# Expert products on two blocks of 768 tokens instead of three of 512

## The reference

```python
def _moe2_ref(x, w_gate, w1, w2) -> np.ndarray:   # x 1536x320, E = 8 experts, F = 1024
    logits = x @ w_gate
    logits = logits - logits.max()
    P = np.exp(logits)
    for _ in range(8):
        P /= P.sum(1, keepdims=True) + 1e-09
        P /= P.sum(0, keepdims=True) + 1e-09
        P *= N / E
    for e in range(E):
        h = np.maximum(x @ w1[e], 0.0)
        ye = h @ w2[e]
        out += P[:, e:e + 1] * ye
    return out
```

## Time and profile before

| | us |
|---|---|
| median of 3 runs | 947.43 |
| the three runs | 945.85, 947.43, 947.50 |
| the profiled execution, its own time | 945.77 |
| its span on the page | 944.1 |
| PE busy | 933.1 (99%) |
| DVE busy | 648.5 (69%) |
| POOL busy | 440.4 (47%) |
| ACT busy | 353.0 (37%) |
| step 0 of the experts starts at | 266.85 |

### The profile page before, as it was taken

One profiled execution on the slowest core, in us unless ns is written; L12 is line 12 of the kernel. 1 busy time (PEld: TensorE's weight loads), 2 busy tenths in 40 slices (PEclk: granted clock), 3 DMA queues, 4 the chain that ended last, 5 costly groups with the idle time before them and its releaser, 6 DMA issues.

```text
span 944.1 us, 16696 instructions
## 1 busy us (share of the span) xinstructions
PE 933.1 (99%) x6519; PEld 889.8 (94%) x6529; DVE 648.5 (69%) x1066; ACT 353.0 (37%) x659; POOL 440.4 (47%) x501
## 2 busy tenths in 40 slices
PE   8999999999999999999999999999999999999998
PEld 5999888888789999999999999999999999999998
DVE  6787555458778899876666766666676666667664
ACT  5664543353453333333322432333243233323221
POOL 4463231057498646465733652573365256336000
PEclk9999999999999999999999999999999999999999
DMA  7980221011011111112111121111112111110000
GB/s 128 216 139 1 78 79 35 1 34 34 1 34 34 35 35 34 35 34 59 44 34 35 37 65 35 32 37 34 35 38 64 35 34 35 35 34 1 28 29 29
DMA packets 82796, 42.39 MB, mean 45 GB/s; under 512 B 54270, under 2 KB 82302, under 8 KB 82718
## 3 DMA queue, kind: packets, MB, share of 16 engines
q1 hardware_dynamic: 82510, 41.23, 17.0%
q10 hardware_dynamic: 208, 0.11, 0.1%
HBM read 39.13 MB, written 2.11 MB: 44 GB/s over the span
## 4 chain that ended last, share of the span: by engine, by line
PE 91%; DVE 6%; ACT 1%; issue 1%; POOL 0%; DVEq 0%; POOLq 0%; ACTq 0%
PE psB L1641 11%; PE psB L1642 11%; PE psB L1643 11%; PE psA L1627 8%; PE psA L1626 8%; PE psA L1625 8%; PE psA L1624 8%; PE psA L1554 8%; PE psB L1473 2%; PE psA L1452 2%; PE psB L1573 2%; PE psB L1575 2%; PE psB L1574 2%; DVE gl L1377 1%; PE psB L1580 1%
## 5 line engine op out<-in xcount | busy, mean ns | idle before, releaser
L676 POOL TENSOR_TENSOR wst<-raw_w,wst 128x128 fp32r<-128x128 f32 (+2 forms) x192 | 163.1, 862 | 304.1 <-ACT wst L891 175.3
L1641 PE MATMUL psB<-w2s,gh 128*128 128x320 f32 x768 | 238.6, 311 | 0.9 <-DVE acc L1351 0.9
L1643 PE MATMUL psB<-w2s,gl 128*128 128x320 f32 x768 | 237.3, 309 | 0.0
L1642 PE MATMUL psB<-w2s,gh 128*128 128x320 f32 x768 | 237.3, 309 | 0.0
L1377 DVE SCALAR_TENSOR_TENSOR gl<-part,gh 128x512 fp32r<-128x512 f32 x192 | 160.5, 876 | 63.4 <-ACT gh L998 62.8
L998 ACT ACTIVATE gh<-part 128x512 fp32r<-128x512 f32 x192 | 110.8, 624 | 245.3 <-DVE part L1371 245.3
L1627 PE MATMUL psA<-xop,wst 96*128 96x256 f32 x672 | 190.2, 283 | 0.0
L1626 PE MATMUL psA<-xop,wst 128*128 128x256 f32 x672 | 190.2, 283 | 0.0
L1625 PE MATMUL psA<-xop,wst 128*128 128x256 f32 x672 | 190.2, 283 | 0.0
L1624 PE MATMUL psA<-xop,wst 128*128 128x256 f32 x672 | 190.0, 283 | 0.0
L1641 PEld LDWEIGHTS psB<-w2s,gh 128*128 128x128 f32 x768 | 144.6, 188 | 1.3 <-DVE gl L1377 1.1
(11 more groups left out here) (193 smaller groups left out, 1377.3 us busy)
## 6 DMA issues: line engine op xcount, KB each, us to landing
raw_w<-in_moe_w_dram SPq DMA_DIRECT2D x32, 320.0 KB, 3.2
raw_w<-in_moe_w_dram SPq DMA_DIRECT2D x32, 256.0 KB, 2.7
raw_w<-in_moe_w_dram SPq DMA_DIRECT2D x96, 64.0 KB, 2.5
qs<-in_q_dram SPq DMA_DIRECT2D x12, 160.0 KB, 3.5
ks<-in_k_dram SPq DMA_DIRECT2D x12, 160.0 KB, 3.7
vz<-in_v_dram SPq DMA_DIRECT2D x12, 160.0 KB, 3.5
og<-in_o_gate_dram SPq DMA_DIRECT2D x12, 160.0 KB, 4.0
out_dram<-acc SPq DMA_DIRECT2D x5, 320.0 KB, 2.3
```

The source lines that it names most:

```text
L676: return pool.tensor_tensor(dst, raw, high.bitcast(F32), ALU.subtract)
L1641: pe.matmul(bank, gh[:, slot, cols], w2[:, f, 0, :], start=first, stop=False)
L1642: pe.matmul(bank, gh[:, slot, cols], w2[:, f, 1, :], start=False, stop=False)
L1643: last = pe.matmul(bank, gl[:, slot, cols], w2[:, f, 0, :], start=False, stop=end)
```

## The change

The experts take two blocks of WB = 768 tokens (halves of HT = 384), so there are 64 steps instead of 96 and a product is four matmuls of 384 columns. The seven products take turns in two banks of `psA`; the second projection has six token tiles, in the other two banks of `psA` and the four of `psB`, and its 36 matmuls are put in six pieces of six between the products. DVE adds each product by itself (six additions, `ADDS` = 6), and the two hidden tiles are finished at different points of the step. Weight slots are five: pair 0 alternates between two, pairs 1 to 3 have one each. The rounds stand at steps 4 to 11. The MLP still works on 512-token blocks; its middle block is half of either expert block, so the pieces of `xop` are 256, 128 and 384 columns a half, and step 0 needs the first two. The order of preparation changes to fit.

```diff
-    PREP = [0, 2, 1, 3]
+    PREP = [0, 1, 2, 3]
-    ROUND_AT = [5, 6, 7, 9, 10, 11, 13, 14]
+    ROUND_AT = [4, 5, 6, 7, 8, 9, 10, 11]
+    TOP_AT, MAX_AT = 2, 3
...
+        product_ps = lambda n, i: psA[:, (NPROD * n + i) % HB, 0:HT]
+        out_ps = lambda j: psA[:, HB + j, 0:DM] if j < HB else psB[:, j - HB, 0:DM]
...
         def slot_of(s, p):
-            return 2 * (s % 2) + p // 2 if p % 2 == 0 else 4 + p // 2
+            return s % 2 if p == 0 else 1 + p
...
# POOL
             pair_low(HALVES, 0)
-            pair_low(HALVES, 2)
-            rest_high(0)
+            kept_high(0)
             main_sums(0)
             main_lows(0)
             main_sums(1)
-            rest_high(1)
+            kept_high(1)
+            main_lows(1)
             pair_low(HALVES, 1)
+            pair_low(HALVES, 2)
+            kept_high(2)
             pair_low(HALVES, 3)
-            main_lows(1)
-            main_sums(2)
-            rest_high(2)
-            pair_low(HALVES + 1, PREP[0])
             main_lows(2)
...
# ACT, middle(n), between keep_first(n) and high_of(n, 0)
+                if n == 0:
+                    pair_s_high(s, 1)
+                    pair_w2_high(s, 2)
+                    pair_w1_high(s, 3)
+                if n == 1:
+                    pair_s_high(s, 2)
+                    x2_rest_high(2)
+                if n == 2:
+                    x2_high(2)
+                    pair_s_high(s, 3)
+                if at == 0 and n > 0:
+                    pair_s_high(s, 1)
+                    both_high(s, 2)
                 if at == 1 and n > 1:
+                    pair_s_high(s, 2)
+                    both_high(s, 3)
+                if at == 2 and n > 2:
                     pair_s_high(s, 3)
+                if s + 1 < STAGES:
+                    if at == 3:
+                        both_high(s + 1, 0)
+                    if at == 4:
+                        pair_s_high(s + 1, 0)
+                    if at == 7:
+                        both_high(s + 1, 1)
...
# DVE, pair(n)
+                if n > 0:
+                    low_of(n - 1, 1)
+                if n == 1:
+                    x2_rest_both(2)
+                    x2_rest_sums(2)
...
+                add(n, 1, part[:, 0, :], part[:, 4, :], 0)
+                if k is not None:
+                    if k == 0:
+                        dve.wait_ge(p_exp, 1)
+                    norm_rows(k)
+                add(n, 2, part[:, 2, :], part[:, 4, :], 0)
+                if p == 1 and blk > 0:
+                    for j in range(4, WT):
+                        read_o(blk - 1, j)
+                if k is not None:
+                    read_columns(k)
+                add(n, 3, part[:, 3, :], part[:, 2, :], 2)
+                if k is not None:
+                    norm_columns(k)
+                add(n, 4, part[:, 1, :], part[:, 3, :], 3)
+                add(n, 5, part[:, 2:4, :], part[:, 2:4, :], 4)
+                low_of(n, 0)
+                add(n, 6, part[:, 2, :], part[:, 2, :], 5)
+                if n == 1:
+                    x2_rest_low(2)
+                    dve.wait_ge(xa, XA * 2 + 1)
+                    sums_of_main(dve, xw, 0, 2)
+                if p == 0 and blk > 0:
+                    if blk == 1:
+                        dve.wait_ge(xl, XL * 3)
+                    for j in range(4):
+                        read_o(blk - 1, j)
...
# PE, pair(n)
+                at_least(pe, added, ADDS * n - 1)
+                product(n, 0, 0, 0)
+                if n == 1:
+                    logits(NTB - 1)
+                at_least(pe, added, ADDS * n)
+                product(n, 1, 1, 2)
+                behind(n, 0)
+                pe.wait_ge(p1_read, n + 1)
+                product(n, 2, 3, 5)
+                behind(n, 1)
+                if k is not None or n == TOP_AT or n == MAX_AT:
+                    pe.wait_ge(added, ADDS * n + 2)
+                if k is not None:
+                    column_sums(k)
+                pe.wait_ge(added, ADDS * n + 1)
+                product(n, 3, 6, 4)
                 behind(n, 2)
+                if k is not None:
+                    pe.wait_ge(sink, SINK_STEPS * k + COLUMNS_READ)
+                pe.wait_ge(added, ADDS * n + 2)
+                product(n, 4, 5, 3)
                 behind(n, 3)
+                pe.wait_ge(added, ADDS * n + 3)
+                product(n, 5, 4, 6)
+                behind(n, 4)
+                pe.wait_ge(added, ADDS * n + 4)
+                product(n, 6, 2, 1)
+                behind(n, 5)
```

More of the change, by code:

```diff
@@ L150, in build @@
         og = asb("og", [P, NU, DM], F32)
+        hh = asb("hh", [P, H, DV], F32)
+        t1 = asb("t1", [P, H, DV], F32)
+        den = asb("den", [P, 2, H], F32)
+        ug = asb("ug", [P, H, D], F32)
+        yy = [asb(f"yy{b}", [P, H, D], F32) for b in range(B)]
         parts = asb("parts", [BH * NC, 2, PARTS, L], BF16)
@@ L373, in hidden_gone @@
         def hidden_gone(s, p):
-            if s == 2 and p % 2 == 0:
+            if s == 2 and p == 0:
                 return g_used, RING + NTB * NF
-            before = s - 2 if p % 2 == 0 else s - 1
+            before = s - 2 if p == 0 else s - 1
             if before < 1:
@@ L561, in _ @@
                     load_pair(s, p)
-            cuts = list(range(0, NT, 2)) + [NT - 1, NT]
-            for t0, t_end in zip(cuts, cuts[1:]):
-                sp.wait_ge(o_read, JT + (E - 1) * NT + t_end)
-                row = (t0 // 2 % B) * NC + t0 // JT * 2 + t0 % 2
-                sp.dma_start(out.rearrange("(t p) d -> p t d", p=P)[:, row:row + t_end - t0, :],
-                             acc[:, t0:t_end, :]).then_inc(stored, 16)
+            cuts = [0]
+            for wb in range(NWB):
+                for h in range(2):
+                    for c, tiles in ((0, 2), (2, 1)):
+                        t0 = (wb * 2 + h) * 3 + c
+                        cuts.append(t0 + tiles)
+                        sp.wait_ge(o_read, WT + (E - 1) * NT + t0 + tiles)
+                        row = wb * NC + 2 + h if c else h * NC + 4 * wb
+                        sp.dma_start(out.rearrange("(t p) d -> p t d", p=P)[:, row:row + tiles, :],
+                                     acc[:, t0:t0 + tiles, :]).then_inc(stored, 16)
             sp.wait_ge(stored, (len(cuts) - 1) * 16)
@@ new lines, in kept_high, with main_lows @@
+            def kept_high(q):
+                pool.wait_ge(xd, XD * q + 6)
+                pool.tensor_copy(xop_of(q, 0)[2 * R32:3 * R32], xraw_of(q, 2)[2 * R32:3 * R32]).then_inc(xp, 1)
+                pool.wait_ge(xp, XP * (q + 1))
+            def main_lows(q):
+                high, low, raw, y0, y1 = xop_of(q, 0), xop_of(q, 1), xraw_of(q, 1), y_of(q, 1), y_of(q, 2)
+                pool.wait_ge(xa, XA * q + 5)
+                low_of(low[:, 0, :], y0[:, 0, :], high[:, 0, :]).then_inc(xl, 1)
+                low_of(low[:, 2:4, :], y1, high[:, 2:4, :]).then_inc(xl, 1)
+                pool.wait_ge(xa, XA * (q + 1))
@@ L1416, in _ @@
             for n in range(NP):
                 pair(n)
-            for j in range(JT):
-                read_o(E * NTB - 1, j)
+            low_of(NP - 1, 1)
+            for j in range(WT):
+                read_o(E * NWB - 1, j)
         @block.tensor
@@ L1731, in _ @@
                 pair(n)
-            for k in range(PP):
-                behind(NP, k)
+            pe.wait_ge(g2, 2 * NP)
+            for j in range(WT):
+                for f in range(2):
+                    expert_out(NP - 1, f, j)
 _INS = ["q", "k", "v", "i_gate", "f_gate", "o_gate", "moe_w_in", "moe_w_out", "moe2_w_gate", "moe2_w1", "moe2_w2"]
```

506 lines of the change are left out of this document (223 added, 283 removed).

## The result

The changed kernel takes 979.34 us (median of four runs, 978.52 to 980.63), the kernel before 946.64 (four runs, 945.85 to 947.50): a ratio of 1.0346, with an interval of 1.0328 to 1.0364. It is slower by 32.7 us where the forecast was 21.7 slower (968, range 949 to 990). The profiled execution has a span of 976.4 us against 944.1.

A forecast was written before the change was run, and what follows sets the result against it. PE, busy 99% of the span, was taken to bound the kernel by matmul count times pace, its waits added in full. Terms -11 + 2 + 13.3 + 7.5 + 4.5 + 3 + 2.4 = +21.7 on 945.8 gave 968 us, range 949 to 990.

The forecast's parts named there:

- Term 1: Matmul pace in all steps: fewer, wider matmuls, 384 columns at 0.174 us each, save 11 us (-13 to -9.5).
- Term 3: First steps: late additions make PE wait 4.0 us (first part, pair 3's weights), then 3.5, 4.8 and 1; +13.3 us.
- Term 4: Rounds, steps 4 to 11: row sums between additions 1 and 2, reads and POOL's disturbance delay PE; +7.5 us.
- Term 5: Block ends: four output reads use up slack, so DVE's waits for POOL count at 7 ends; +4.5 us (0 to 12).
- Term 6: Steps 3 and 7: POOL's `w2` subtraction is in the way of tile 0's low part; +3 us (0 to 8).
- Rival E: Clock: PE's rests in steps 1 and 2 drop it to 1.2 GHz, 10 us each, 998 us; above 985, chance 0.10.
- Term 2: Kernel's end: the last pieces wait for the last step's addition 6, ReLU and low part; +2.0 us (1.5 to 2.5).
- Term 7: After the rounds: POOL's scaling of `acc` makes pair 0 of expert 2 late, ACT waiting ahead of a ReLU; +2.4 us.

The follow-up runs named there:

- g1: Changed kernel with ACT casting pair 3's raw weights after step 0's second ReLU, not ahead of the first: 977.22 us, ratio 1.0322.
- f4: Changed kernel with POOL preparing no weights from pair 1 of the second expert on, only counting semaphores: 959.92 us, ratio 1.0138.
- g3: Changed kernel with POOL's subtractions of 640 columns cut into four and those of 512 into two: 963.62 us, ratio 1.0182.
- f3: Changed kernel with two of a block end's four output reads moved ahead of addition 5: 977.85 us, ratio 1.0333.
- f1: Changed kernel with unused matmuls filling PE's waits in steps 1, 2, 8, 9 and 10: 976.07 us, ratio 1.0312.
- j1: Changed kernel with row sums moved, start spread, POOL's subtractions and scaling cut, two early reads, ACT's pair 0 cast after both ReLUs: 951.03 us, ratio 1.0051.

## Why the prediction was right, and where it was short

- **Direction and mechanism.** What was named decided: two banks leave a slack of 0.5 and 1.3 us at each step's end, and everything that stands in the chain of low part, ReLU and addition is added. The additions that PE waits for, the times (addition 1 of step 1 ends at 290.0 forecast, 290.7 measured) and the wait at the end (2.0 and 1.79) came out. The total is 11.3 us beyond the forecast. That it still lies in the range is in part luck: the clock makes up 5.3 to 9.2 of these 11.3, and its size was not worked out from anything.
- **Term 1** was mis-sized by the choice between two neighbours' lines: 0.174 was taken, 0.175 measured. The other line (0.1748) was right.
- **Term 3's first part** had 4.0 us before step 1's second product, and PE waited 0.59 and 0.83. One cause is a misreading of the earlier trace rows: the 2.82 us of logits are one block's, and it took half of them. In step 1 the logits take 2.82 again, so PE wanted the addition 1.5 us later than forecast from that alone. The other is that pair 3's weights landed at 278.54 and not at 279.9, and the addition ended at 282.0 and not 283.3. The later parts took it over: 5.24 for 3.5 and 4.18 for 4.8. The sum of waits nearly held (11.5 for 13.3) while the places did not: where PE waited less at first, DVE was as late as forecast one product on. g1 shows how little the DMA and the cast weigh: 1.7 us in its trace.
- **Term 4**, without the clock, came to 7.5 as forecast, by luck: three errors cancel. The order of DVE was priced at 4.2 and costs 2.0 (f4). The 2.6 us that `column_sums` itself takes in eight rounds, and the 3.9 that the rounds cost in the kernel before, were not reckoned. POOL was priced at 3.5, and takes 16.5 - 4.6 - 5.1 = 6.8. The step that failed is this last price. Its only rows for an instruction held by POOL were low parts; the row sums are small instructions, of which two in a row can each be held for about 1 us. Steps 8 to 10 lose 9.6 in f4, 4.5 of it in waits and 5.1 by the clock.
- **Term 5** had the right places, nearly the size (4.5, 5.2) and the right account. With POOL idle in f4, addition 1 of step 25 ends 3.2 us into the step (forecast 3.4), PE wants it at 3.86, and nothing waits; f4 and g3 took POOL's long instructions away and the waits went. What it did not foresee is f3: 0.9 us less of reads in the chain gains nothing where the low part then meets the start of a POOL instruction.
- **Term 6** was wrong in its place (no wait in the steps it named) and right in size by luck; the same subtraction of 1.57 us met the low part of tile 1 instead, in the step behind a block end (26, 34 and so on), 3.2 us.
- **Rival E** was given as one thing, ten microseconds for each of three rests. It came in small, in five places: 9.2 us of matmul time, of which f1 and g1 get 5.3 back, about half of what the forecast lacked. That it stood as a rival and at nothing in the sum is the step that failed most: the forecast's own waits of 3.5 and 4.8 us in steps 1 and 2 called for a term.
- **Term 2** holds. **Term 7** has its size (2.4, 2.7) and, in the main, its cause: in step 12 ACT's cast of pair 0's sums starts at 434.54, when POOL has them, with a ReLU behind it, and without this order step 13 is quiet in j1. A low part held by POOL for some 0.8 us (1.73) stands behind the ReLU, and is part of the same wait.
